# The expert stage's input rows: turned by VectorE from a block stored two ahead, in place of transposes on TensorE

## The reference

```python
# 1: linear attention with decay, 8 heads of 64
state = gamma * state + k_t (outer) v_t;  y_t = scale * q_t @ state
# 2: x = y as (B, S, 512)
h = relu(x @ w_in); gate = sigmoid(conv3(h)); x2 = (h * gate) @ w_out      # 512 -> 1024 -> 512
# 3: each token goes to one of 8 experts
e = argmax(x2 @ w_gate), or the expert of the token before where a local gate is shut
out = softmax(x2 @ w_gate)[e] * (relu(x2 @ w1[e]) @ w2[e])                 # 512 -> 1024 -> 512
```

## Time and profile before

| what | value |
|---|---|
| median of three runs | 418.8 us |
| the profiled execution | 419.02 us |
| its span, first to last instruction | 416.9 us |
| TensorE, mean granted clock | 0.997 |
| TensorE products busy | 405.5 us, 97% |
| VectorE busy | 228.8 us, 55% |
| ScalarE busy | 209.7 us, 50% |
| GpSimd busy | 105.1 us, 25% |
| DMA, mean | 162 GB/s |

### The profile page before, as it was taken

The page is one execution under the profiler, slowest core; times in us unless marked ns, Lnnn a source line. Parts: engine busy times, 40 slices in busy tenths (PEclk is TensorE's granted clock), DMA queues, the critical chain, the costliest instruction groups (busy, mean ns, idle before and its releaser), DMA issues.

```text
span 416.9 us, 7057 instructions
## 1 busy us (share of the span) xinstructions
PE 405.5 (97%) x2597; PEld 342.1 (82%) x2598; DVE 228.8 (55%) x293; ACT 209.7 (50%) x293; POOL 105.1 (25%) x104
## 2 busy tenths in 40 slices
PE   7999999999999999999999999999999999999992
PEld 3888799887889987879788888888888888888881
DVE  4788739973004879477376511106961273655640
ACT  2334678670214865380557423327852563747640
POOL 3344873000000000026622212213232222322320
PEclk9999999999999999999999999999999999999998
DMA  8999900000520007753474711015691173572500
GB/s 291 406 412 415 396 6 2 0 2 0 201 91 12 2 0 314 292 192 109 169 290 150 328 50 50 26 50 201 269 416 54 44 307 155 181 291 64 222 17 25
DMA packets 16152, 67.74 MB, mean 162 GB/s; under 512 B 2623, under 2 KB 4159, under 8 KB 11776
## 3 DMA queue, kind: packets, MB, share of 16 engines
q1 hardware_dynamic: 12928, 58.87, 35.9%
q0 software_dynamic: 2912, 8.13, 5.7%
q10 hardware_dynamic: 288, 0.41, 0.3%
HBM read 58.49 MB, written 10.22 MB: 165 GB/s over the span
## 4 chain that ended last, share of the span: by engine, by line
PE 92%; DMA 5%; SPq 1%; ACT 1%; issue 0%; POOL 0%; DVE 0%; POOLq 0%; ACTq 0%
PE ps L996 26%; PE ps L998 25%; PE ps L997 25%; DMA kv<-qkv 5%; PE ps L1262 4%; PE ps L1236 2%; PE ps L1047 2%; PE ps L1044 2%; PE ps L1026 1%; PE ps L1093 1%; PE ps L1010 1%; PE ps L1072 0%; PE ps L1168 0%; PE ps L1102 0%; PE ps L1159 0%
## 5 line engine op out<-in xcount | busy, mean ns | idle before, releaser
L929 DVE TENSOR_TENSOR hT<-ps,hT 128x512 fp32r<-128x512 f32 x34 | 23.5, 691 | 88.5 <-ACT hT L643 88.5
L916 DVE TENSOR_TENSOR wx<-raw_w,wx 128x1024 fp32r<-128x1024 f32 x56 | 65.1, 1218 | 2.8 <-ACT wx L584 1.6
L996 PE MATMUL ps<-wx,hT 128*128 128x512 f32 x136 | 56.1, 413 | 0.3 <-issue 0.3
L584 ACT CAST wx<-raw_w 128x1024 fp32r<-128x1024 f32 x56 | 55.0, 1049 | 0.0
L996 PE MATMUL ps<-wx,xT 128*128 128x512 f32 x136 | 54.7, 402 | 0.2 <-DVE xT L952 0.2
L998 PE MATMUL ps<-wx,xT 128*128 128x512 f32 x136 | 53.2, 391 | 0.0
L998 PE MATMUL ps<-wx,hT 128*128 128x512 f32 x136 | 53.1, 391 | 0.0
L997 PE MATMUL ps<-wx,xT 128*128 128x512 f32 x136 | 53.0, 390 | 0.0
L997 PE MATMUL ps<-wx,hT 128*128 128x512 f32 x136 | 53.0, 390 | 0.0
L996 PE MATMUL ps<-x,win 128*128 128x384 f32 x128 | 43.2, 337 | 0.0
L998 PE MATMUL ps<-x,win 128*128 128x384 f32 x128 | 42.8, 334 | 0.0
(11 more groups left out here) (162 smaller groups left out, 760.0 us busy)
## 6 DMA issues: line engine op xcount, KB each, us to landing
raw_w<-w_exp SPq DMA_DIRECT2D x28, 1024.0 KB, 4.7
qk<-qkv SPq DMA_DIRECT2D x7, 768.0 KB, 9.7
raw_first<-w_exp SPq DMA_DIRECT2D x4, 1024.0 KB, 8.0
kv<-qkv SPq DMA_DIRECT2D x4, 768.0 KB, 11.5
x_rows<-x2n SPq DMA_DIRECT2D x11, 256.0 KB, 2.8
kv<-qkv SPq DMA_DIRECT2D x7, 384.0 KB, 10.2
x_early<-x2n SPq DMA_DIRECT2D x10, 256.0 KB, 2.3
win_raw<-w_in SPq DMA_DIRECT2D x4, 512.0 KB, 12.2
```

The costliest lines, as they stand in the source:

```text
L584: nc.scalar.copy(wx[:, slot, 0, c], raw).then_inc(wx_hi[w], 1)
L916: nc.vector.tensor_tensor(wx[:, slot, 1, c], raw, wx[:, slot, 0, c].bitcast(F32), ALU.subtract).then_inc(w2_lo_dve if w else w1_lo_dve, 1)
L929: nc.vector.tensor_tensor(lo, psHT[:, 512 * a:512 * a + 512], hi.bitcast(F32), ALU.subtract).then_inc(hT_done, 1)
L996: mm(o, lh, rl, start=first, stop=False)
```

## The change

For blocks 1 and on, TensorE no longer transposes the input rows. SyncE gets a `step` of its own in each block: it waits for the gather of block g+2 and for VectorE's turn of block g+1, stores `xg` to a block in DRAM (`x_block`), waits for that, and loads it in four DMAs to `xq`, so that each quarter of 32 partitions holds 128 of the 512 columns, with the rows in four groups of 32. VectorE turns this with one 32x32 transpose instruction of 128x512 (`turn_x`) to `xF` in SBUF. ScalarE and VectorE split x from `xF`, no longer from PSUM, and after the second half of the hidden rows. The gather now waits for the store of `xg`, one block further ahead, and stands before the scatter. SyncE's loads of weights are placed among these steps.

The rows of x then stand in another order on the partitions (32q + i holds column 128q + 32k + i). The host orders w1 so (`quarters`), and block 0, which still comes from TensorE, is made in that order: each transpose or product onto 128 columns becomes four products onto 32. For the same reason the halves of x2's last tile are now every other 64 columns (`column_half`), and stored so.

Further: `three` can have the transposes of the hidden rows between its first and second product (`amid`), the first one product into k = 1 of the second half in the first layer, the second one product into k = 1 of the second layer. One piece of block 0's weights goes from GpSimd to VectorE, and the first block of an expert has ReLU before the evacuation on ScalarE.

```diff
 WPE = 8
+TR = 32
+NQ = P // TR
 KEEP_ABOVE = -1.5 * 2.0 ** -23
...
 def build(nc, qkv, w_in, conv_w, w_out, w_out_t, w_gl, w_exp, decay_c, const_c, first_c, out):
...
     x2_early = nc.dram_tensor("x2_early", (T - 2 * P, DM), F32, kind="Internal").ap()
+    x_block = nc.dram_tensor("x_block", (P, DM), F32, kind="Internal").ap()
     KB = 1024
...
     hs = at("hs", [P, FF], F32, 140)
+    xF = at("xF", [P, KD, P], F32, 192)
+    xq = at("xq", [P, NQ, P], F32, 196)
     os_ = at("os", [P, DM], F32, 194)
...
 psEnd, psRow, psSlot, psInv = bank(6), bank(3), bank(7), bank(2)
-psP1, psHT, psXT, psO = bank(0, 2), bank(2, 2), bank(4), bank(5)
+psP1, psHT, psO = bank(0, 2), bank(2, 2), bank(5)
+def column_half(a, n):
+    return a.rearrange("t (q n c) -> t n q c", q=NQ, n=2)[:, n]
...
     for n in range(2):
-        h = slice(DM // 2 * n, DM // 2 * n + DM // 2)
         sp.wait_ge(x2_out, TT + n)
-        sp.dma_start(x2_rows[T - P:T, h], x2n[:, (TT - 1) % 3, h]).then_inc(x2_stored[(TT - 1) % 3], 16)
+        sp.dma_start(column_half(x2_rows[T - P:T, :], n), column_half(x2n[:, (TT - 1) % 3, :], n)
+                     ).then_inc(x2_stored[(TT - 1) % 3], 16)
         if n == 0:
...
             raw(1, 1, raw_w2, raw_w2_in, (0,))
-    sp.wait_ge(x2_done, TT + 1)
-    sp.wait_ge(gathered, 32)
-    raw(1, 1, raw_w2, raw_w2_in, (1,))
-    raw(0, 2, raw_w1[0], raw_w1_in[0])
-    sp.wait_ge(w2_lo_pool, 3)
+    def step(g):
+        sp.wait_ge(gathered, 16 * g + 48)
+        sp.wait_ge(x_turned, 16 * g + 48)
+        sp.dma_start(x_block, xg[:]).then_inc(x_stored, 16)
+        sp.wait_ge(x_stored, 16 * g + 32)
+        for q in range(NQ):
+            sp.dma_start(xq[TR * q:TR * q + TR],
+                         x_block[:, P * q:P * q + P].rearrange("(b j) n -> j b n", j=TR)
+                         ).then_inc(quartered, 16)
     def raw_w2_next(e):
...
     def raw_w1_next(e, s):
-        sp.wait_ge(w1_lo_dve, 4 * e - 5)
-        raw(0, e, raw_w1[s], raw_w1_in[s])
-    with sp.Fori(2, E - 2, 2) as ee:
-        raw_w2_next(ee)
-        raw_w1_next(ee + 1, 1)
-        raw_w2_next(ee + 1)
-        raw_w1_next(ee + 2, 0)
-    raw_w2_next(E - 2)
-    raw_w1_next(E - 1, 1)
-    raw_w2_next(E - 1)
+        sp.wait_ge(w1_lo_dve, 4 * e + 7)
+        raw(0, e + 3, raw_w1[s], raw_w1_in[s])
+    sp.wait_ge(x_first, 2)
+    step(-1)
+    sp.wait_ge(x2_done, TT + 1)
+    raw(1, 1, raw_w2, raw_w2_in, (1,))
+    step(0)
+    raw(0, 2, raw_w1[0], raw_w1_in[0])
+    sp.wait_ge(w2_lo_pool, 2)
+    def expert(e, s, ahead):
+        first, end = block_range(sp, e)
+        if not (isinstance(e, int) and e == 0):
+            if ahead > 0:
+                raw_w2_next(e + 1)
+            step(first)
+        rest(sp, first, end, step)
+        if ahead > 2:
+            raw_w1_next(e, 1 - s)
+    sp.wait_ge(tables, 1)
+    expert(0, 0, 3)
+    with sp.Fori(1, E - 4, 2) as ee:
+        expert(ee, 1, 3)
+        expert(ee + 1, 0, 3)
+    expert(E - 3, 1, 2)
+    expert(E - 2, 0, 1)
+    expert(E - 1, 1, 0)
 @block.gpsimd
 def _(pool):
-    pool.sem_inc(xg_free, 1)
...
     def gather(g):
-        pool.wait_ge(xg_free, g + 1)
         nc.gpsimd.tensor_copy(gnow[:], gidx[:, bass.ds(g, 1)]).then_inc(g_copied, 1)
...
     def step(g):
+        pool.wait_ge(x_stored, 16 * g + 16)
+        gather(g + 2)
         scatter_before(g)
-        pool.wait_ge(gathered, 16 * g + 32)
-        gather(g + 2)
     def wide(a):
...
     pool.wait_ge(gathered, 16)
-    pool.wait_ge(xg_free, 2)
+    pool.wait_ge(xg_read, 1)
     nc.gpsimd.tensor_copy(gnow[:], gidx[:, 1:2]).then_inc(g_copied, 1)
...
         xg[:], None, x2_rows, bass.IndirectOffsetOnAxis(gnow[:, 0:1], 0)).then_inc(gathered, 16)
-    weights_lo(1, 0, 0, (1, 2))
+    weights_lo(1, 0, 0, (1,))
     pool.wait_ge(tables, 1)
-    pool.wait_ge(gathered, 32)
+    pool.wait_ge(x_stored, 16)
     gather(2)
     def expert(e):
...
-    def x_hi(g):
-        act.wait_ge(xg_free, g + 2)
-        nc.scalar.copy(xT[:, 0].rearrange("p k t -> p (k t)"), psXT).then_inc(xT_hi, 1)
+    def x_hi():
+        nc.scalar.copy(xT[:, 0].rearrange("p k t -> p (k t)"), xF[:].rearrange("p k t -> p (k t)")).then_inc(xT_hi, 1)
     def h_hi(g, a):
...
         relu(g, 1)
-        x_hi(g + 1)
         h_hi(g, 1)
+        act.wait_ge(x_turned, 16 * g + 48)
+        x_hi()
     def first_step(g, e, slot):
+        relu(g, 0)
         evac_before(g, o_done)
-        relu(g, 0)
+        h_hi(g, 0)
         if e is not None:
             weights_hi(0, e, slot, (3,))
-        h_hi(g, 0)
         relu(g, 1)
-        x_hi(g + 1)
         h_hi(g, 1)
+        act.wait_ge(x_turned, 16 * g + 48)
+        x_hi()
...
         act.wait_ge(x2_done, TT + n)
-        h = slice(DM // 2 * n, DM // 2 * n + DM // 2)
-        nc.scalar.copy(x2n[:, (TT - 1) % 3, h], psXh[n]).then_inc(x2_out, 1)
+        nc.scalar.copy(column_half(x2n[:, (TT - 1) % 3, :], n),
+                       psXh[n].rearrange("t (q c) -> t q c", q=NQ)).then_inc(x2_out, 1)
         act.wait_ge(x_first, n + 1)
...
     relu(0, 1)
-    x_hi(1)
     h_hi(0, 1)
+    act.wait_ge(x_turned, 48)
+    x_hi()
     weights_hi(0, 1, 1, (2, 3))
     def expert(e, s, ahead):
...
 @block.vector
 def _(dve):
-    dve.sem_inc(w2_lo_dve, 3)
+    dve.sem_inc(w2_lo_dve, 2)
+    dve.sem_inc(x_turned, 32)
     nc.vector.memset(warm[:], 0.0).then_inc(made, 1)
...
+    def turn_x(g):
+        dve.wait_ge(quartered, 64 * g)
+        nc.vector.transpose(xF[:].rearrange("p k (q t) -> p k q t", q=NQ),
+                            xq[:].rearrange("p q (k i) -> p k q i", k=KD)).then_inc(x_turned, 16)
     def x_lo(g):
         dve.wait_ge(xT_hi, g + 1)
-        nc.vector.tensor_tensor(xT[:, 1].rearrange("p k t -> p (k t)"), psXT,
+        nc.vector.tensor_tensor(xT[:, 1].rearrange("p k t -> p (k t)"), xF[:].rearrange("p k t -> p (k t)"),
                                 xT[:, 0].rearrange("p k t -> p (k t)").bitcast(F32),
...
     def step(g):
         h_lo(g, 0)
+        turn_x(g + 1)
+        h_lo(g, 1)
         x_lo(g + 1)
-        h_lo(g, 1)
     def first_step(g, e, slot):
         h_lo(g, 0)
+        turn_x(g + 1)
         if e is not None:
             weights_lo(0, e, slot, (3,))
+        h_lo(g, 1)
         x_lo(g + 1)
-        h_lo(g, 1)
...
                                 ALU.subtract).then_inc(x0_lo if n == 0 else xT_done, 1)
+    weights_lo(1, 0, 0, (2,))
     h_lo(0, 0)
+    h_lo(0, 1)
+    turn_x(1)
     x_lo(1)
-    h_lo(0, 1)
     weights_lo(0, 1, 1, range(4))
     def expert(e, s, ahead):
...
-    def three(o, lh, ll, rh, rl, first, last):
+    def three(o, lh, ll, rh, rl, first, last, amid=None):
         mm(o, lh, rl, start=first, stop=False)
+        if amid:
+            amid()
         mm(o, ll, rh, start=False, stop=False)
...
     def x2_half(n, k):
         ts = slice(S - P, S)
-        ws = slice(DM * k + DM // 2 * n, DM * k + DM // 2 * n + DM // 2)
-        last = three(psXh[n], hg[:, 0, k, ts], hg[:, 1, k, ts], wout[:, 0, ws], wout[:, 1, ws],
+        wh, wl = (column_half(wout[:, w, DM * k:DM * k + DM], n) for w in range(2))
+        last = three(psXh[n].rearrange("t (q c) -> t q c", q=NQ), hg[:, 0, k, ts], hg[:, 1, k, ts], wh, wl,
                      k == 0, k == KF - 1)
...
         for k in parts:
-            ins = mm(psX0[:, k, :], x2n[:, t % 3, P * k:P * k + P], oh0[:, t - TT + 2, :], start=False,
-                     stop=True, skip_group_check=True)
+            for q in range(NQ):
+                ins = mm(psX0[TR * q:TR * q + TR, k, :], x2n[:, t % 3, P * q + TR * k:P * q + TR * k + TR],
+                         oh0[:, t - TT + 2, :], start=False, stop=True, skip_group_check=True)
             if t == TT - 1 and k % 2 == 1:
...
         for k in range(KD):
-            last = nc.tensor.transpose(psX0[:, k, :], xg[:, P * k:P * k + P], ident)
-        last.then_inc(xg_free, 1)
+            for q in range(NQ):
+                last = mm(psX0[TR * q:TR * q + TR, k, :], xg[:, P * q + TR * k:P * q + TR * k + TR], ident,
+                          start=True, stop=True)
+        last.then_inc(xg_read, 1)
...
                         inverse()
-    def turn_x(g):
-        pe.wait_ge(gathered, 16 * g + 16)
-        for k in range(KD):
-            last = nc.tensor.transpose(psXT[:, P * k:P * k + P], xg[:, P * k:P * k + P], ident)
-        last.then_inc(xg_free, 1)
     def first_w1():
...
         pe.wait_ge(w1_lo_dve, 3)
-        for k, a in ((0, 0), (0, 1), (1, 0), (1, 1), (2, 0), (3, 0), (2, 1), (3, 1)):
-            if (k, a) == (1, 0):
+        for k, a in ((0, 0), (0, 1), (1, 0), (2, 0), (3, 0), (1, 1), (2, 1), (3, 1)):
+            if (k, a) == (0, 1):
                 last_rows(TT - 1, TT + 1, (2, 3))
...
-    def w1_part(a, k, slot):
+    def w1_part(a, k, slot, amid=None):
...
         last = three(o, xT[:, 0, k, :], xT[:, 1, k, :], wx[:, slot, 0, c], wx[:, slot, 1, c],
-                     k == 0, k == KD - 1)
+                     k == 0, k == KD - 1, amid)
```

(25 more changed lines are left out.)

6 lines of the change are left out of this document (4 added, 2 removed).

## The result

The changed kernel takes **422.15 us** (median of 10 runs, 420.09 to 423.35), the kernel before, run beside it, 418.97 (10 runs, 418.48 to 419.65). The ratio is **1.0068**, 95% interval 1.0052 to 1.0084: slower by 0.7%, little but clear of the noise, where the forecast was 415.1, or 0.991. The profiled execution took 422.28.

The account below looks back on a forecast made before the run. TensorE, busy 97% of the span, was taken as the bound. Terms -7.8 + 0.5 + 1.2 + 1.7 + 0.7 = -3.7 from the profiled 419.02, less 0.2 for the median, gave 415.1 us; range 412.5 to 418.0.

Parts of the forecast that it names:

- Transposes off TensorE: Input rows of blocks 1 and on: seventeen groups of four transposes leave TensorE at 0.46 us each, -7.8 us.
- Hidden transposes in new places: Two moved groups per block: hidden rows are ready 1.10 us after the half's last product, covered by 1.135, cost 0.
- Rival E: Steady blocks: a gap per block replaces the group, as if the 0.03 margin were missed by 0.1; +3.2, 418.3, chance 0.05.
- Block 0's 96 records: Block 0's input rows: products onto 32 columns overlap 4 abreast, so 96 records take 2.7 us, +0.5.
- rival C: Block 0's rows: products on 32 columns don't overlap, +8.3 in place of +0.5, 422.9 us; chance 0.05.
- Path of block 1: Start of block 1: x now goes through store, gather, loads and VectorE's turn, so it starts at 214.05; +1.2 us.
- Queue behind VectorE's turn: Block 1: six weight subtractions behind the turn delay the hidden rows' subtraction, TensorE waits to 221.65; +1.7 us.
- One short expert: Expert 2's single block 7: seven casts and subtractions run into block 8 and delay hT's subtraction; +0.7 us.
- Steady blocks, costed at nothing: Steady blocks: the next x arrives with about 5 us to spare, 2.7 of it used behind weights; cost 0.
- Rival D: Changes of expert: the store of x sits behind weights beyond the 5 us, say 0.8 at each of six; 419.9, chance 0.05.

Follow-up runs that it names:

- the last run above: The changed kernel with weight loads spread one matrix per step of x, plus block 1's weights split partly ahead of its x: 418.56 us, ratio 0.9986.

## Why the prediction was wrong

By its own steps:

- **Transposes off TensorE, -7.8.** Right: clean blocks take 11.81 to 11.87, 0.4 to 0.5 less than before (12.28).
- **Hidden transposes in new places, 0.** Right, the margin of 0.03 held: clean blocks show no wait at them. Rival E was wrong.
- **Block 0's 96 records, +0.5.** Right: 32 take 1.08 as shown, and the next group starts 0.89 later, 0.028 a record, four abreast against the 0.11 of a single one. All 96 take 3.0 (forecast 2.7), and TensorE is done with block 0 at 212.9, as forecast. The logits were the right row to go by; rival C was wrong.
- **Path of block 1, +1.2.** Right: block 1 starts at 214.06, forecast 214.05, TensorE waiting 1.03 for VectorE's x. That it is right to 0.01 is luck: the store took 2.0 and not 2.5, the loads 3.3 (3.2), the turn 0.70 (0.69), and from the turn to TensorE's start, over ScalarE's cast and VectorE's subtraction, it took 2.3 where 2.1 was taken. The second half-store, in 256 B pieces, landed 2.2 after its issue where the one in 1 KB pieces took 1.7, 0.5 more (taken 0.4), 0.2 of it in the issue itself (0.53 against 0.32). The Trainium skill ("DMA: Bandwidth & Descriptors", Specifications) wants 512 B or more for line rate; the prediction's estimate from it was 0.3 more, and the trace agrees that such a store is slower, by somewhat more than that.
- **Queue behind VectorE's turn, +1.7.** Nearly: block 1 took 13.28, 1.5 over a clean one.
- **One short expert, +0.7.** Right, but visible only with the weights out of the way: 12.62 and 12.63 are 0.8 over a clean block.
- **"Steady blocks, costed at nothing": the step that failed.** The three long blocks are 7.7 too long (3.0 + 2.8 + 1.9); less the 0.8 of the short expert, which the forecast had, it measured 6.9, where the forecast had 0. With it the sum is 422.0, and 422.15 was measured. Rival D had a part of the mechanism, the late store of x, at 0.8 a change of expert and a chance of 0.05. The measured time lies nearest to rival C's 422.9, but that is chance, C's mechanism did not happen.

In that step four things went wrong. *The size of the burst*: "four of them are some 10 us of traffic" was worked out from 4.7 for one. The bytes do take about that, but the last of them landed 15.6 after the first issue. DMA over 18 us, sampled in 40 slices, of the changed kernel and of the one before (busy share in tenths, GB/s):

```profile
DMA  4544917999999999998999999999998941000000
GB/s 137 157 129 138 291 55 291 400 437 419 364 373 428 437 364 346 373 410 373 460 437 410 455 419 419 437 437 419 437 400 355 391 164 18 0 18 18 0 0 0
```
```profile
DMA  0009569899999999899999999999983000000391
GB/s 0 0 0 164 109 200 419 364 473 400 437 382 400 437 346 455 310 401 391 428 451 391 492 382 473 382 473 382 410 355 128 27 27 0 0 0 0 127 391 64
```

The DMA engines are full at some 410 GB/s for about 11 us in both. The burst filled the engines just as long before; the kernel before had no chain of small transfers that had to get through it. *The time of issue*: taken at -1.4 to +0.2 from the block's start. That held for three of the five bursts (-1.1), and two of these cost nothing. In block 2 it was +2.5 for w1 and +5.0 and later for w2, and in block 8 +3.7, because SyncE first had to wait for x, and w1 now stood ahead of w2. So in block 2 the burst ended 18 us into the cycle, not 9. *The gather*: the store of x was to be asked for 6.3 into the block; it was asked for 9.8 in (237.11 against 227.34), since the gather itself took 7.7 beside the weights. *What waits*: I looked only at the store of x. That w2 itself, needed 8.6 us into the block, would be late was not asked at all, and it made the larger part: ScalarE's cast stands ahead of the ReLU in its order, so a late weight stops the block at once. The scatter too was put at nothing; in the changed kernel that cost nothing, in the last run above it did.

The rest of the sum, 415.1, was right within 0.7, as the run without weight bytes (415.82) shows. What makes a small transfer wait beside weights, the shared bandwidth or the order of completions, stays open.

## What to carry to other kernels

Moving work from a busy engine to transfers turns a slack of bandwidth into a matter of latency: before doing it, write down for each transfer in the new chain, and for each that it may push back, when it is asked for, when it is due, and how long everything asked for before it occupies the DMA engines, on any queue. Add up a burst from the first issue to the last landing in the trace, not from the median of one load. And where large prefetches and a short chain share the DMA engines, ask for one matrix at a time between two steps of the chain, and let the ones with slack go early.
